# V read straight from its input by chunk, exponentials written in V's row order, in an attention and mixture-of-experts kernel

## The reference

```python
def _attn_ref(q, k, v, mem_k, mem_v):          # 4 batches, 8 heads, 768 rows, 64 wide; 8 memory rows
    chunk, left_ctx, right_ctx = (32, 16, 8)
    for c in range(nc):
        l_start = max(0, c_start - left_ctx)
        r_end = min(S, c_end + right_ctx)
        k_full = np.concatenate([mem_k, k[:, :, l_start:r_end]], axis=2)
        v_full = np.concatenate([mem_v, v[:, :, l_start:r_end]], axis=2)
        scores = scale * np.matmul(q_c, k_full.transpose(0, 1, 3, 2))
        scores = scores - np.max(scores, axis=-1, keepdims=True)
        a = np.exp(scores)
        a = a / (np.sum(a, axis=-1, keepdims=True) + 1e-09)
        out[:, :, c_start:c_end] = np.matmul(a, v_full)

x = attn_out as (3072, 512)
x = ((x @ w_a) * (x @ w_b)) @ w_out            # 512 -> 1536 -> 512
P = exp(x @ w_gate - max), 8 rounds of row and column scaling
out = sum over 8 experts of P[:, e] * (relu(x @ w1[e]) @ w2[e])    # 512 -> 1024 -> 512
```

## Time and profile before

| | |
|---|---|
| time, median of 3 runs | 2740.11 us (2739.94 to 2742.03) |
| time of the profiled execution | 2741.23 us |
| span of the profiled execution | 2739.5 us |
| attention, quads 0 to 23 | the first 196 us |
| PE busy | 2662.7 us, 97% of the span |
| DVE, ACT, POOL busy | 51%, 28%, 19% |
| instruction queue (q8) | 121 packets, 1.98 MB |
| matmuls and weight loads of PE | 15264 each |

### The profile page before, as it was taken

One profiled execution on the slowest core, in us unless ns is written; L12 is line 12 of the kernel. 1 busy time (PEld: TensorE's weight loads), 2 busy tenths in 40 slices (PEclk: granted clock), 3 DMA queues, 4 the chain that ended last, 5 costly groups with the idle time before them and its releaser, 6 DMA issues.

```text
span 2739.5 us, 36851 instructions
## 1 busy us (share of the span) xinstructions
PE 2662.7 (97%) x15264; PEld 2196.0 (80%) x15264; DVE 1388.3 (51%) x2039; ACT 770.8 (28%) x1301; POOL 516.0 (19%) x440
## 2 busy tenths in 40 slices
PE   7779999999999999999999999999999999999999
PEld 6667878878777888888888888888888888888887
DVE  2454554454558454454564554544546544545544
ACT  3444332232333333333332221222222212222211
POOL 0036520020254545545430000000001000000000
PEclk8899999999999999999999999999999999999999
DMA  9946553433355565555545334333333443343342
GB/s 217 194 112 242 218 190 145 162 141 139 146 173 173 196 207 173 203 200 177 209 153 199 128 131 165 127 140 156 127 149 147 158 159 137 127 168 128 131 165 89
DMA packets 138454, 445.23 MB, mean 163 GB/s; under 512 B 34608, under 2 KB 94000, under 8 KB 106800
## 3 DMA queue, kind: packets, MB, share of 16 engines
q1 hardware_dynamic: 138288, 442.88, 45.9%
HBM read 315.97 MB, written 133.43 MB: 164 GB/s over the span
## 4 chain that ended last, share of the span: by engine, by line
PE 92%; DVE 3%; issue 2%; POOL 1%; ACT 1%; DMA 0%; DVEq 0%; ACTq 0%; POOLq 0%
PE bank L729 44%; PE bank L804 44%; PE bank L651 2%; PE bank L666 1%; PE bank L691 1%; PE bank L678 1%; POOL X L572 1%; DVE tmp L1232 1%; PE bank L701 0%; DVE Y L1265 0%; DVE Y L1323 0%; ACT X L987 0%; DVE hid L1328 0%; DVE hid L1384 0%; PE bank L706 0%
## 5 line engine op out<-in xcount | busy, mean ns | idle before, releaser
L729 PE MATMUL bank<-X,W 128*128 128x512 f32 x5550 | 1397.1, 390 | 14.8 <-ACT tmp L1035 4.9
L729 PEld LDWEIGHTS bank<-X,W 128*128 128x128 f32 x5550 | 1040.1, 188 | 240.4 <-issue 20.6
L804 PE MATMUL bank<-W,hid 128*128 128x512 f32 x4608 | 1153.7, 389 | 2.4 <-DVE Y L1262 2.4
L804 PEld LDWEIGHTS bank<-W,hid 128*128 128x128 f32 x4608 | 864.5, 188 | 182.3 <-DVE Y L1262 2.8
L1262 DVE SCALAR_TENSOR_TENSOR Y<-bank,gate,Y 128x512 f32<-128x512 f32 x720 | 539.7, 750 | 567.8 <-PE bank L804 560.4
L572 POOL TENSOR_TENSOR X<-Y,X 128x1024 fp32r<-128x1024 f32 x30 | 77.9, 2599 | 1025.1 <-ACT X L987 1025.0
L1093 ACT ACTIVATE hid<-tmp 128x512 fp32r<-128x512 f32 x192 | 121.3, 632 | 354.7 <-DVE tmp L1229 274.6
L804 PE MATMUL bank<-hid,W 128*128 128x512 f32 x864 | 219.5, 390 | 1.2 <-issue 1.2
L1031 ACT ACTIVATE tmp<-bank 128x512 f32<-128x512 f32 x132 | 78.8, 597 | 487.1 <-PE bank L729 487.1
L1384 DVE SCALAR_TENSOR_TENSOR hid<-bank,hid 128x512 fp32r<-128x512 f32 x192 | 132.7, 691 | 162.9 <-ACT hid L1093 162.8
L804 PEld LDWEIGHTS bank<-hid,W 128*128 128x128 f32 x864 | 162.4, 188 | 35.5 <-issue 1.6
(11 more groups left out here) (85 smaller groups left out, 1062.5 us busy)
## 6 DMA issues: line engine op xcount, KB each, us to landing
W<-w_kept SPq DMA_DIRECT2D x88, 1792.0 KB, 8.7
w_kept<-W SPq DMA_DIRECT2D x44, 1792.0 KB, 6.7
W<-w_kept SPq DMA_DIRECT2D x76, 1024.0 KB, 4.9
w_kept<-W SPq DMA_DIRECT2D x38, 1024.0 KB, 4.9
raw<-in_moe_w_dram SPq DMA_DIRECT2D x64, 512.0 KB, 6.4
Kr<-in_k_dram SPq DMA_DIRECT2D x12, 512.0 KB, 6.1
Qr<-in_q_dram SPq DMA_DIRECT2D x12, 512.0 KB, 7.8
Vw<-v_rows SPq DMA_DIRECT2D x48, 128.0 KB
```

The costliest lines, as they stand in the source:

```text
L729: last = nc.tensor.matmul(into[:, :], W1[:, c % 2, ws, w_slot, kc, :], X[:, pos, xs, kc, :], start=(start and kc == 0 and n == 0), stop=(k ...
L804: last = nc.tensor.matmul(into[:, :], lhsT, rhs, start=(j == 0 and n == 0), stop=(j == 1 and n == 2))
```

## The change

`v_rows` and its copies are gone. `load_v(r)` reads V's input itself, one transfer for each f and chunk: 56 sequence rows of four heads, in pieces of 256 bytes (64 numbers). The first chunk of a batch has 40 rows and a transfer of 16 more, the last one 48 rows and a transfer of 8 more, to fill the tile. The memory's eight rows are loaded only for the first three quads of a batch (`g < VS`), which fills each slot once. VS goes from 4 to 3. `vm_rows` of all batches is written at the start, and SP waits for it ahead of the first `load_v`. A chunk's keys now stand in V's order, 56 of the sequence and then 8 of the memory: DVE writes the differences into a new tile Df, and `exps` takes them to Pr in three activations that put the columns in that order. The differences of quad r wait for the exponentials of quad r - 1, as Df has one buffer.

```diff
-    VS = 4
+    VS = 3
...
+            Df = sb("Df", [P, HP, 2, KEYS], F32, first)
...
+        def loads_v(r):
+            return sum((12, 10, 10, 8, 8, 10)[i % G] for i in range(r % VS, r + 1, VS))
...
             def load_v(r):
                 b, g, slot = r // G, r % G, r % VS
                 if r >= VS:
                     sp.wait_ge(a_o, r - VS + 1)
-                if b > 0:
-                    sp.wait_ge(s_vr[TH - 1 + b], 16 * 8)
-                elif g in (0, 1, 3):
-                    sp.wait_ge(s_vr[(g + 1) // 2], 16 * (6, 2, 4)[(g + 1) // 2])
                 for f in range(2):
-                    into = Vw[64 * f:64 * f + 64, slot].rearrange("p c h d -> p c (h d)")
-                    of = v_rows[b, f, g * QUAD:g * QUAD + QUAD, :].rearrange("(c s) n -> s c n", s=CHUNK)
-                    sp.dma_start(into[0:CHUNK], of).then_inc(s_v[slot], 16)
-                    of = v_rows[b, f, g * QUAD + CHUNK:(g + 1) * QUAD + CHUNK, :].rearrange("(c s) n -> s c n", s=CHUNK)
-                    sp.dma_start(into[BLK:KEYS], of[0:KEYS - BLK]).then_inc(s_v[slot], 16)
-                    sp.dma_start(into[CHUNK:BLK],
-                                 vm_rows[b, f].unsqueeze(1).to_broadcast([MEM, 4, HP * HD])).then_inc(s_v[slot], 16)
+                    for c in range(4):
+                        start = g * QUAD + c * CHUNK - LEFT
+                        s0, s1 = max(start, 0), min(start + WIN, S)
+                        at = 64 * f + s0 - start
+                        sp.dma_start(Vw[at:at + s1 - s0, slot, c],
+                                     v[b, f::2, s0:s1, :].rearrange("h s d -> s h d")).then_inc(s_v[slot], 16)
+                        if s0 > start:
+                            sp.dma_start(Vw[64 * f:at, slot, c],
+                                         v[b, f::2, 0:LEFT, :].rearrange("h s d -> s h d")).then_inc(s_v[slot], 16)
+                        if s1 < start + WIN:
+                            sp.dma_start(Vw[64 * f + s1 - start:64 * f + WIN, slot, c],
+                                         v[b, f::2, S - RIGHT:S, :].rearrange("h s d -> s h d")).then_inc(s_v[slot], 16)
+                    if g < VS:
+                        sp.dma_start(Vw[64 * f + WIN:64 * f + KEYS, slot].rearrange("p c h d -> p c (h d)"),
+                                     vm_rows[b, f].unsqueeze(1).to_broadcast([MEM, 4, HP * HD])).then_inc(s_v[slot], 16)
...
             load_q(0, 0)
-            rows_third(0)
+            for b in range(B):
+                for f in range(2):
+                    sp.dma_start(vm_rows[b, f].rearrange("m (h d) -> m h d", h=HP),
+                                 mem_v[b, f::2].rearrange("h m d -> m h d")).then_inc(s_vm, 16)
             load_k(0, 1)
-            rows_third(1)
+            sp.wait_ge(s_vm, 16 * 2 * B)
             load_v(0)
...
-            rows_third(2)
...
-            rows_batch(1)
...
                 if b < B and g == 3:
-                    rows_batch(b)
                     load_k(b, 1)
...
             def exps(r):
                 act.wait_ge(a_sub, 2 * r + 2)
-                nc.scalar.activation(Pr[:, r % 2], Pr[:, r % 2], ACT.Exp).then_inc(a_exp, 1)
+                if r > 1:
+                    act.wait_ge(a_pt, r - 1)
+                    act.wait_ge(a_sum, r - 1)
+                d, p = (t.rearrange("p h f n -> p (h f) n") for t in (Df[:, :, :, :], Pr[:, r % 2]))
+                nc.scalar.activation(p[:, :, 0:CHUNK], d[:, :, 0:CHUNK], ACT.Exp)
+                nc.scalar.activation(p[:, :, CHUNK:WIN], d[:, :, BLK:KEYS], ACT.Exp)
+                nc.scalar.activation(p[:, :, WIN:KEYS], d[:, :, CHUNK:BLK], ACT.Exp).then_inc(a_exp, 1)
...
             def differences(r):
-                if r > 1:
-                    dve.wait_ge(a_pt, r - 1)
+                if r > 0:
+                    dve.wait_ge(a_exp, r)
                 for f in range(2):
                     dve.wait_ge(a_mx, 2 * r + f + 1)
-                    nc.vector.tensor_tensor(Pr[:, r % 2, :, f, :],
+                    nc.vector.tensor_tensor(Df[:, :, f, :],
```

More of the change, by code:

```diff
@@ L131, in build @@
         w1_kept = nc.dram_tensor("w1_kept", [2 * V1 + V2, P, 4 * NP * P], F32).ap()
-        v_rows = nc.dram_tensor("v_rows", [B, 2, LEFT + S + 2 * RIGHT, HP * HD], F32).ap()
         vm_rows = nc.dram_tensor("vm_rows", [B, 2, MEM, HP * HD], F32).ap()
@@ L149, in build @@
         s_v = [sem(f"s_v{i}") for i in range(VS)]
-        s_vr = [sem(f"s_vr{i}") for i in range(TH + B - 1)]
+        s_vm = sem("s_vm")
         s_zero = sem("s_zero")
@@ L354, in load_mem @@
                 sp.dma_start(Mk[:, :, :], mem_k[b].rearrange("h m d -> m h d")).then_inc(s_mk, 16)
[L357 to L371, removed]
             def load_v(r):
@@ L582, in clear @@
                 else:
-                    none, base, sign = p[:, :, KEYS - RIGHT:KEYS], QUAD - CHUNK - 1, -1
+                    none, base, sign = p[:, :, WIN - RIGHT:WIN], QUAD - CHUNK - 1, -1
                 nc.gpsimd.affine_select(out=none, in_=none, compare_op=ALU.is_ge, fill=0.0, base=base,
@@ L682, in weigh_v @@
                 pe.wait_ge(a_ptc, r + 1)
-                pe.wait_ge(s_v[r % VS], 6 * 16 * (r // VS + 1))
+                pe.wait_ge(s_v[r % VS], 16 * loads_v(r))
                 if r > 0:
```

## The result

| | before | changed |
|---|---|---|
| median of the runs | 2740.03 us (2739.83 to 2742.03, 4 runs) | 2723.88 us (2719.9 to 2726.73, 4 runs) |
| ratio to before | | 0.9938 [0.9921, 0.9956] |
| profiled execution, its span | 2741.2, 2739.5 us | 2725.75, 2723.8 us |

The changed kernel is faster by 0.6%, 16 us. The forecast was 2719, in a range from 2700 to 2741.

What follows compares the result with a forecast made beforehand. Program fetches standing behind data in the DMA engines were taken to bound the attention stage: 2741.2 - 28 + 2.5 (late Q) + 1.5 (start) + 1.4 (exponentials) = 2719 us, in a range from 2700 to 2741.

Steps and rivals of the forecast that it cites:

- The bound: Attention stage, quads 1 to 17: PE stops because fetches of its program stand behind data in the DMA engines, 5.97 us a piece.
- The rival "no change": Attention stage: PE's fetches stay as late, or extra DVE and ACT steps eat the gain; 2735 to 2746 us, chance 0.14.
- The bytes: DMA in quads 1 to 17: 28.0 MB fall to 22.0 MB, as copies to `v_rows` and some V loads go.
- I take a third of the excess as left: 4.8 us, 115 us: Quads 1 to 17: each of 24 program pieces between 4.15 us, every fetch in time, and 5.97; 28 us gained from 143.5.
- 2.5 + 1.5 + 1.4: Losses in us booked apart: late Q of batch 3, later Q at the start, exponentials in the first four quads.
- The last third of Q: Batch 3, quad 17: Q issued behind twelve V transfers lands at 161, needed at 158.51; loss 2.5 us, or 5.5.
- the start: Kernel start: memory's V copies, their wait and V of quad 0 delay the second third of Q; loss 1.5 us.
- Issue on SP: SP's queue: V transfers at 0.4 us each, bound 0.7; 3.6 us a quad, at most 6.0, hidden behind 6.4.
- Pieces of 256 bytes: V's loads into SBUF: 18.2 ns a piece, 31 as bound; 1792 pieces a quad take 2.0 or 3.5 us.
- The rival "slower": V's loads: a 256-byte piece costs like a big one, slower from 57 ns on; 2754 us at 62 ns, chance 0.11.
- Exponentials: ACT: three activations take 0.34 us more a quad, hidden but in the first four quads, 1.4 us in all.
- Three slots: V's buffer: loads wait one quad later, but V is used 19 us on against some 12 for issue and landing; hidden.

## Why the prediction came out as it did

**The bound was named rightly.** With the copies out and nothing else, the ratio is the change's. With the copies back it is lost, but there mostly to late data. The bytes (21.9 MB against 22.0) and the rest that stays as it was came as worked out; the clock is 0.90, where "above 0.9" was said, and 5.5 of the 16.8 us come by way of it. The rival "no change" falls with the stops, 32.3 to 15.4 us, though "about 10" was forecast. The Trainium skill (Runtime: NRT & Kernel Launch, Instruction fetch mechanics) would have the boundary mostly hidden; in this trace it is not, even with hardly any V loaded (14.5 us).

**The step that was mis-sized is "I take a third of the excess as left: 4.8 us, 115 us".** The window took 126.7 us, outside the 110 to 120 named. Of this 5.6 us are waits for Q and K and about 1.6 us the lower clock behind the longest. For losses of this kind the forecast booked 2.5 + 1.5 + 1.4 apart. Without these 7.2 us it is 126.7 - 7.2 = 119.5 us, 4.5 above the 115; and the kernels with the last third of Q, and then with both, moved forward measure 121.4 and 120.4. A piece of program thus takes 5.0 us, not 4.8. The reason is the part of a fetch that doesn't depend on load. I had taken 4.15 us, the quickest pieces of the earlier trace rows, as what every piece takes if data are out of the way. Those two pieces end in stops of only 0.24 and 0.30 us, so their length is nearly all PE's own work, and 24 of them, 100 us, are the stretch with hardly a stop. With V's loads gone it takes 113.8 us, a mean of 4.7 us a piece, and without its 14.5 us of stops it would be 99.3. My 10 us of stops lay below what can be reached by cutting V alone.

**The last third of Q** stopped PE at the place forecast, in quad 17, for 4.1 us instead of 2.5. From SP's first transfer of V behind `weigh_v(15)` to the point where PE wanted Q there were 7.85 us (128.07 to 135.92) where the earlier trace rows gave 7.3. Q's landing took 5.3 us, 5 had been taken. Twelve transfers took 6.7 us instead of 4.8, and this is the term that was off. To it comes the lower clock behind the stop, 1.6 us, which no term held. Moving Q forward gave 3.3 to 5.3 us back in the profiles. At **the start**, the other of the two waits for Q is 4.9 - 4.1 = 0.8 us, against 1.5 forecast.

**Issue on SP.** Over all 192 transfers of V the median was as forecast, but not in loaded stretches. By line (ns min/median/max), and one quad at 28.54 us:

```profile
L371 SPq DMA_DIRECT2D Vw<-in_v_dram x192: 282/419/1975, 9.8 to 166.5; - x192
```

```profile
28.54 5.83 SPq L371 DMA_DIRECT2D Vw<-in_v_dram  x8
```

0.42 us at the median, 0.73 in that quad. The bound of 0.7 that "would make it wrong" was met in places and hidden there, since a quad takes 126.7 / 17 = 7.5 us.

**Pieces of 256 bytes.** From 156 to 160 us the changed kernel moves, beside one packet of program, nothing but V:

```profile
q1 hardware_dynamic: 1695, 0.41, 46.2%
```

0.462 x 16 x 4 us / 1695 = 17.4 ns a piece; 18.2 was taken, 31 was the bound and 57 the point at which it turns slower. The rival "slower" falls. The Trainium skill's rule against transfers under 64 KB (DMA: Bandwidth & Descriptors, Rules for kernel authors) is not borne out here by 56 KB transfers: the kernel with only the copies removed, whose transfers of V into SBUF are of 128, 96 and 32 KB, has the ratio 0.9942 against 0.9938.

**Exponentials:** 0.40 us a quad instead of 0.34, and no cost that the experiment shows. **Three slots:** called hidden. They are not free and not a loss: with them the stops are shorter and the waits for data longer, and both kernels, with copies and without, come out nearly even (0.9986 to 1 and 0.9938 or 0.9927 to 0.9924).

In sum: forecast 28 us in the stretch less 5.4 of costs, 22; measured 16.8 in the stretch with the costs in it, and 15.7 at the end.

## What to carry to other kernels

If an engine stops inside a loop that has no wait, at a constant count of its instructions, look at when the packets of its instruction queue move: bytes that no engine waits for can be what delays them, and taking them out pays. Not every "issue" is such a stop: where it stands ahead of an instruction that waits on a semaphore, off that count, look for a landing of data. How much can be had is read from what a whole fetch takes from one boundary to the next when it is quick, 3.5 us here, set against what the shortest stretch of program between two boundaries takes, 2.5 us. When one transfer becomes many, look at what stands behind them on the issuing queue and move what is used soonest ahead, which took the ratio here from 0.9938 and 0.9927 to 0.9907, at the edge of what the intervals tell apart.

## What the runs showed of the hardware that was not expected

- PE went on 1.2 to 1.7 us after the packet with its next 16 KB had ended, behind a queue at a DMA share of 110% (kernel before) as behind one that had just run dry (without V). The packet itself took 0.9 to 1.7 us. Stops of 14.5 us were left at a share of 0.45. Why the lag is that long no run shows.
- With the blocks of K and Q halved, PE stopped 9.0 us at boundaries instead of 21.0, while its waits for data rose from none to 14.7. What sets the delay of a single packet, beyond the load as a whole, stays open.
- Six copies inside DRAM held SP for 10.03 us, 1.67 each, at a DMA share of 0.75; the median of the kernel before is 0.69.
- After 4.1 us of idle PE the next 32 matmuls took 3.68 us, at the lower clock, instead of 2.04: this stop cost 1.6 us more than its length. Length alone does not decide: in the same kernel 16 matmuls took 1.98 us, at a granted clock of 0.50, after a wait of 0.77 us at 19.22, and 1.14 us after a wait of 0.73 us at 132.97.
